# Gated linear attention and a two-stage mixer on one core: where the last two of six transpositions stand, and in which order ACT copies them

## What is computed

```python
m_new = max(f[t] + m, i[t]);  f_stab = exp(f[t] + m - m_new);  i_stab = exp(i[t] - m_new)
C = f_stab * C + i_stab * outer(v[t], k[t]);  n = f_stab * n + i_stab * k[t]
y[t] = sigmoid(o[t]) * (C @ q[t]) / max(abs(n @ q[t]), 1.0)
```

```python
h = relu(x.T @ w_tok1) @ w_tok2        # 768 -> 256 -> 768, over tokens
u = x + h.T
out = u + relu(u @ w_ch1) @ w_ch2      # 320 -> 1536 -> 320, over channels
```

## Time and profile before

| | us |
|---|---|
| median of 3 runs | 486.13 |
| lowest, highest | 482.44, 488.3 |
| the profiled execution, its own time | 481.5 |
| its span | 479.8 |
| PE, DVE, ACT, POOL busy | 451.7, 285.9, 227.6, 157.4 |

### The profile page before, as it was taken

How to read it: one execution, slowest core, us unless ns; L and a number is a source line. 1 busy time by engine, 2 the same in 40 slices (tenths; PEclk the granted TensorE clock), 3 DMA queues, 4 the chain that set the end, 5 groups by cost and what they waited for, 6 DMA issues and landing times.

```text
span 479.8 us, 9414 instructions
## 1 busy us (share of the span) xinstructions
PE 451.7 (94%) x3408; PEld 414.7 (86%) x3408; DVE 285.9 (60%) x660; ACT 227.6 (47%) x564; POOL 157.4 (33%) x212
## 2 busy tenths in 40 slices
PE   5988998788999999899999999899999999999996
PEld 3665787678999999789999999789999998899996
DVE  7476877777787425588787325587797324412312
ACT  2634557865655225865665125766555212212111
POOL 3424232546655001366655002266654000000000
PEclk9998799899999999999999999899999999999999
DMA  7499897224444302344454301344431001000101
GB/s 215 138 256 268 238 286 262 71 79 135 135 141 138 103 1 63 95 135 133 135 149 131 103 10 59 88 134 136 134 103 43 1 1 42 1 0 1 42 0 41
DMA packets 39189, 50.91 MB, mean 106 GB/s; under 512 B 3554, under 2 KB 31016, under 8 KB 39144
## 3 DMA queue, kind: packets, MB, share of 16 engines
q1 hardware_dynamic: 39144, 50.32, 35.2%
HBM read 46.27 MB, written 4.03 MB: 105 GB/s over the span
## 4 chain that ended last, share of the span: by engine, by line
PE 80%; ACT 6%; DVE 6%; issue 3%; DMA 3%; SPq 1%; POOL 0%; DVEq 0%; ACTq 0%; POOLq 0%
PE pC L952 30%; PE pA L1024 6%; PE pA L1025 6%; PE pA L1026 6%; PE pS L872 6%; PE pA L952 4%; PE pY L929 4%; PE pA L1028 3%; PE pA L1029 3%; DMA qd<-qT_dram 3%; PE pY L910 3%; PE pN L886 2%; PE pC L840 1%; DVE wc_lo L679 1%; PE pY L919 1%
## 5 line engine op out<-in xcount | busy, mean ns | idle before, releaser
L813 DVE SCALAR_TENSOR_TENSOR h_lo<-pA,h_hi 128x384 fp32r<-128x384 f32 x96 | 53.2, 554 | 119.0 <-ACT h_hi L615 119.0
L615 ACT ACTIVATE h_hi<-pA 128x384 fp32r<-128x384 f32 x96 | 46.7, 486 | 132.8 <-PE pA L1029 132.8
L952 PE MATMUL pC<-wc_hi,h_hi 128*128 128x320 f32 x288 | 94.0, 326 | 0.1
L952 PE MATMUL pC<-wc_lo,h_hi 128*128 128x320 f32 x288 | 89.0, 309 | 0.0
L952 PE MATMUL pC<-wc_hi,h_lo 128*128 128x320 f32 x288 | 88.6, 308 | 0.0
L422 POOL TENSOR_TENSOR gb<-gb,pb 128x384 f32<-128x384 f32 (+1 forms) x54 | 46.5, 862 | 112.1 <-ACT pb L529 111.9
L519 ACT ACTIVATE gb<-gb,aT 128x128 f32<-128x128 f32 x192 | 63.0, 389 | 14.3 <-POOL gb L433 14.3
L1024 PE MATMUL pA<-uT_hi,wc_hi 128*128 128x384 f32 x192 | 65.7, 342 | 2.5 <-DVE uT_hi L791 2.5
L1025 PE MATMUL pA<-uT_lo,wc_hi 128*128 128x384 f32 x192 | 65.0, 339 | 0.0
L1026 PE MATMUL pA<-uT_hi,wc_lo 128*128 128x384 f32 x192 | 64.7, 337 | 0.0
L952 PEld LDWEIGHTS pC<-wc_hi,h_hi 128*128 128x128 f32 x288 | 54.3, 189 | 0.9 <-issue 0.4
(11 more groups left out here) (113 smaller groups left out, 871.1 us busy)
## 6 DMA issues: line engine op xcount, KB each, us to landing
gb<-g_dram SPq DMA_DIRECT2D x23, 512.0 KB, 3.9
kv<-kvN_dram SPq DMA_DIRECT2D x24, 324.0 KB, 4.9
kd<-kT_dram SPq DMA_DIRECT2D x24, 180.0 KB
qz<-qT_dram SPq DMA_DIRECT2D x72, 60.0 KB
out_dram<-u SPq DMA_DIRECT2D x24, 160.0 KB, 1.9
gq<-g_dram SPq DMA_DIRECT2D x60, 60.0 KB
qd<-qT_dram SPq DMA_DIRECT2D x20, 180.0 KB, 5.1
x<-o_gate_dram SPq DMA_DIRECT2D x4, 640.0 KB, 4.5
```

The source lines that it names most:

```text
L615: nc.scalar.activation(h2[0][:, slot % 2], pA[slot % 2][:, 0:HALF], ACT.Relu).then_inc(h2_hi, 1)
L813: nc.vector.scalar_tensor_tensor(h2[1][:, slot % 2], pA[slot % 2][:, 0:HALF], 0.0, h2[0][:, slot % 2].bitcast(F32), ALU.max, ALU.subtract) ...
L952: ins = mm(dst, a[p], b[q], start=first and n == 0, stop=last and n == 2)
```

## The change

The last two transpositions (tiles 4 and 5) go to `pC[0]` and `pC[1]` instead of `pA`, and stand in slot 0: that of tile 4 behind the hidden product, that of tile 5 behind step 2 of the attention. Slots 0 and 1 wait for the low parts of tiles 2 and 3 only; the first `project` waits for all six. PE makes the second token product of tiles 0 to 2 with the piece `m` as the outer loop. Transposition 0 stands ahead of the products of tile 3, transposition 1 behind them, 2 behind tile 4's, and 3 behind tile 5's and step 1 of the attention.

ACT makes the high copy of tile `s - 2` behind its instruction for `u_twice` of tile `s`, where before it was that of tile `s - 1`. Step 1 of the attention moves behind tile 5 on all three engines. Relu of slot 0 stands ahead of the exponentials of step 3. The two last high copies, these exponentials, the start of the next tile (`chunk_start`) and `sigmoid` come between relu of slot 0 and that of slot 1. On DVE `p_low` of step 0 stands behind the low parts of tile 3, and the low parts of tiles 4 and 5 in slot 0.

```diff
...
@@ -148,6 +147,10 @@
         def scores_bank(ba, m):
             return [pS, pC[0], pC[1]][m % NG] if ba == 0 else pS
+
+        def transposed_bank(s):
+
+            return pA[s % 2] if s < NC - 2 else pC[s - (NC - 2)]
         def values_bank(ba, c):
@@ -589,23 +592,21 @@
                     nc.scalar.activation(h1[0][:, m], pA[m][:, 0:DM], ACT.Relu).then_inc(h1_hi, 1)
                 if more:
                     attention(b + 1, 0)
-                for s in range(NC + 1):
-                    if s < NC:
-                        act.wait_ge(u_ready, NC * b + s + 1)
-                        nc.scalar.activation(u[:, s, DM:3 * L], u[:, s, 2 * L:DM], ACT.Copy).then_inc(u_twice, 1)
-                    if s == 0:
-                        continue
-                    s -= 1
+                def u_high(s):
                     act.wait_ge(uT_mm, NC * b + s + 1)
-                    src = pA[s % 2][:, 0:3 * L].rearrange("p (t s) -> p t s", t=3)
+                    src = transposed_bank(s)[:, 0:3 * L].rearrange("p (t s) -> p t s", t=3)
                     nc.scalar.activation(uh[:, :, s * L:(s + 1) * L], src, ACT.Copy).then_inc(uT_hi, 1)
-                    if more and s + 1 == SECOND_AT:
-                        attention(b + 1, 1)
+
+                for s in range(NC):
+                    act.wait_ge(u_ready, NC * b + s + 1)
+                    nc.scalar.activation(u[:, s, DM:3 * L], u[:, s, 2 * L:DM], ACT.Copy).then_inc(u_twice, 1)
+                    if 2 <= s < NC - 1:
+                        u_high(s - 2)
                 if more:
-
+                    attention(b + 1, 1)
+                u_high(NC - 3)
+                if more:
                     p_middle(b + 1, AHEAD - 1)
-                    exps(b + 1, NG)
-                    chunk_start(b + 1, 1)
                 for slot in range(SLOTS):
                     k = SLOTS * b + slot
@@ -616,10 +617,17 @@
                     if b == 0:
                         for n in slot_pieces(slot):
                             split_hi(n)
-                    if more and slot == 0:
-                        sigmoid(b + 1)
+                    if slot == 0:
+                        u_high(NC - 2)
+                        if more:
+                            exps(b + 1, NG)
                     if more:
                         attention(b + 1, slot + AHEAD)
+                    if slot == 0:
+                        u_high(NC - 1)
+                        if more:
+                            chunk_start(b + 1, 1)
+                            sigmoid(b + 1)
             for b in range(B):
                 batch(b, b < B - 1)
@@ -786,9 +794,10 @@
                 def u_low(s):
...
+                    bank_s = transposed_bank(s)
+                    nc.vector.tensor_tensor(ul[:, :, cols], bank_s[:, 0:2 * L].rearrange("p (t s) -> p t s", t=2),
...
-                    nc.vector.tensor_tensor(uh[64:128, 2, cols], pA[s % 2][64:128, 2 * L:3 * L],
...
                 if more:
@@ -798,14 +807,13 @@
                     if b != 0:
                         dve.wait_ge(out_done[s // ST], 16 * ST * b)
                     nc.vector.tensor_tensor(u[:, s, 0:DM], pC[s % ST][:, 0:DM], x[:, s], ALU.add).then_inc(u_ready, 1)
-                    if s >= 2:
+                    if 2 <= s < NC - 1:
                         u_low(s - 2)
-                    if more and s == SECOND_AT:
-                        attention(b + 1, 1)
+                if more:
+                    attention(b + 1, 1)
+                u_low(NC - 3)
                 if more:
                     p_low(b + 1, 0)
-                for s in range(NC - 2, NC):
-                    u_low(s)
                 for slot in range(SLOTS + 1):
                     k = SLOTS * b + slot
                     if slot < SLOTS:
@@ -813,11 +821,15 @@
                         nc.vector.scalar_tensor_tensor(h2[1][:, slot % 2], pA[slot % 2][:, 0:HALF], 0.0,
                                                        h2[0][:, slot % 2].bitcast(F32),
                                                        ALU.max, ALU.subtract).then_inc(h2_lo, 1)
+                    if slot == 0:
+                        u_low(NC - 2)
                     if b == 0:
                         for n in slot_pieces(slot):
                             split_lo(n)
                     if more and slot < SLOTS:
                         attention(b + 1, slot + AHEAD)
+                    if slot == 0:
+                        u_low(NC - 1)
                     if slot == NJ or slot == SLOTS:
                         half = slot // NJ - 1
                         dve.wait_ge(c2_mm, SLOTS * b + slot)
@@ -974,38 +986,46 @@
                 def transposes(s):
+                    bank_s = transposed_bank(s)
                     pe.wait_ge(u_ready, NC * b + s + 1)
-                    if s >= 2:
+                    if s < 2:
+                        pe.wait_ge(h1_lo, MT * b + s + 1)
+                    elif s < NC - 2:
                         pe.wait_ge(uT_lo, 2 * (NC * b + s - 1))
-                    else:
-                        pe.wait_ge(h1_lo, MT * b + s + 1)
...
                     pe.wait_ge(u_twice, NC * b + s + 1)
...
                 if more:
                     attention(b + 1, 0)
-                for s in range(NC):
-                    if s < ST:
-                        if b != 0:
-                            pe.wait_ge(out_ready, 2 * ST * b)
-                    else:
-                        pe.wait_ge(u_ready, NC * b + s - ST + 1)
+                def mixed(s, m):
+
+                    return split_products(pC[s % ST][:, 0:DM], [w[:, m, s * L:(s + 1) * L] for w in wt2],
+                                          [a[:, m] for a in h1], m == 0, m == MT - 1)
+
+                if b != 0:
+                    pe.wait_ge(out_ready, 2 * ST * b)
+                for m in range(MT):
+                    pe.wait_ge(h1_lo, MT * b + m + 1)
+                    if b == 0:
+                        pe.wait_ge(w_lo, 2 + m + 1)
+                    for s in range(ST):
+                        ins = mixed(s, m)
+                        if m == MT - 1:
+                            ins.then_inc(t2_mm, 1)
+                transposes(0)
+                for s in range(ST, NC):
+                    pe.wait_ge(u_ready, NC * b + s - ST + 1)
                     for m in range(MT):
-                        if s == 0:
-                            pe.wait_ge(h1_lo, MT * b + m + 1)
-                            if b == 0:
-                                pe.wait_ge(w_lo, 2 + m + 1)
-                        ins = split_products(pC[s % ST][:, 0:DM], [w[:, m, s * L:(s + 1) * L] for w in wt2],
-                                             [a[:, m] for a in h1], m == 0, m == MT - 1)
+                        ins = mixed(s, m)
                     ins.then_inc(t2_mm, 1)
-                    if s >= 1:
-                        transposes(s - 1)
-                    if more and s == SECOND_AT:
-                        attention(b + 1, 1)
-                transposes(NC - 1)
+                    if s < NC - 1:
+                        transposes(s - 2)
+                if more:
+                    attention(b + 1, 1)
+                transposes(NC - 3)
                 def hidden(slot):
@@ -1014,7 +1034,9 @@
                     cols = slice(half * HALF, (half + 1) * HALF)
                     f = slice(j * L, (j + 1) * L)
                     if slot < 2:
-                        pe.wait_ge(uT_lo, 2 * (NC * b + NC - 1 + slot))
+                        pe.wait_ge(uT_lo, 2 * (NC * b + ST + slot))
+                    if half == 1 and j == 0:
+                        pe.wait_ge(uT_lo, 2 * NC * (b + 1))
                     if slot >= 2:
                         pe.wait_ge(h2_lo, k - 1)
                     if b == 0 and half == 0 and j % 6 == 0:
@@ -1033,6 +1055,8 @@
                     half, j = divmod(slot, NJ)
                     k = SLOTS * b + slot
                     pe.wait_ge(h2_lo, k + 1)
+                    if j == 0 and half == 0:
+                        pe.wait_ge(uT_lo, 2 * NC * (b + 1))
                     if j == 0 and half == 1:
                         pe.wait_ge(out_ready, 2 * ST * b + ST)
                     if b == 0 and half == 0 and j % 2 == 0:
@@ -1045,8 +1069,12 @@
                 for slot in range(SLOTS + 1):
                     if slot < SLOTS:
                         hidden(slot)
+                    if slot == 0:
+                        transposes(NC - 2)
                     if more and slot < SLOTS:
                         attention(b + 1, slot + AHEAD)
+                    if slot == 0:
+                        transposes(NC - 1)
                     if slot >= 1:
                         project(slot - 1)
```

7 lines of the change are left out of this document (3 added, 4 removed).

## The result

The changed kernel took 495.9 us (median of 4 runs, 493.69 to 497.0), the kernel before 484.28 beside it (480.46 to 488.3). The ratio is 1.0271, with a 95% interval of 1.0217 to 1.0325: **slower by 2.7%**, as forecast. The forecast was 495.0, in a range of 482 to 501.

The account below looks back on a forecast made before the run. PE, with 80% of the chain, was taken to bound the kernel, time being won or lost in its waits at the borders. Delays of 4.2 + 2.9 + 1.6 + 0.1 = 8.8 us on a 486.13 median gave 495.0, range 482 to 501.

Parts of the forecast that it names:

- The ring: Loop over tiles: each addition from tile 3 on waits for an older tile's high copy; 2.01 us a tile, before 1.22.
- The wait of PE for `p_low` in slot 0: Second border, after slot 0's hidden product: PE waits some 2 us for p_low, needed for step 2's values.
- The chain to relu of slot 1: ACT's and DVE's work up to relu of slot 1: 4.2, 2.9 and 1.6 us later at the first three borders.
- That a delay there is passed on in full: Behind slot 2's wait PE is busy without a gap, so 4.2, 2.9 and 1.6 us count whole at three borders.
- half clock: Rival: PE falls to half clock more often, 1.6 us behind each of three borders, 499.7 us; chance 0.16.
- The last part, where I forecast 0.1: Last border, no attention: nine products cover h1's low half, the ring costs 2.4; first project 0.1 us later.
- the 8.8 of the sum: Delays at the four borders added: 4.2 + 2.9 + 1.6 + 0.1 = 8.8 us.
- the first two rivals: Ring does not bind and banks help, 480.9 us, chance 0.14; ACT's queue does not reach PE, 487, chance 0.22.
- The first: Rival: ring does not bind, banks remove PE's waits at second, third and last border; 5.2 us gain, 480.9; chance 0.14.

Follow-up runs that it names:

- ring open: Changed kernel with ACT's high copy of tile s - 1, not s - 2, behind u_twice of tile s; 487.08 us, ratio 1.0084 to the kernel before.
- the fillers: Changed kernel with products that nobody reads put into PE's waits at the borders; 494.8 us, ratio 1.0194 to the kernel before.
- the banks alone: Kernel before with transpositions of tiles 4 and 5 into pC and fewer waits, all instructions in their old place; 477.7 us, ratio 0.9890; again 478.58, 0.9880.
- moving one call: Changed kernel with only the sigmoid moved ahead of step 2 of the attention; 491.84 us, ratio 1.0158 to the kernel before.
- ring and step 1 mended: Changed kernel with high copy of s - 1, step 1 back behind tile 3, and here the sigmoid ahead of step 2; 483.12 us, ratio 0.9959.
- step 1 back: Changed kernel with step 1 of the next attention back behind tile 3 on PE, ACT and DVE; 491.81 us, ratio 1.0154 to the kernel before.
- ring with step 1: Changed kernel with high copy of s - 1 behind u_twice of s and step 1 back behind tile 3; 485.13 us, ratio 1.0095.
- PE's order: Kernel before with the banks and the change's PE order up to tile 5, transpositions 4 and 5 right behind tile 5; 481.25 us, ratio 0.9981.

## Why the prediction was right

**The ring.** Forecast 2.01 us a tile, measured 1.98; slot 0 8.9 behind the first product, measured 9.1. I had put the first product of before at 184.26 by counting back from the earlier trace rows, while it starts at 183.96: from there my forecasts are 9.2 for slot 0 and 19.5 for relu of slot 1 (measured 19.54). Opening the ring took 6.3 us of 11.5 away, about 1.0 of it clock at the last border. The wait of PE for `p_low` in slot 0 came too (1.73 us, some 2 forecast), but it is step 0's values that it holds up and not step 2's, as I wrote. The Trainium skill, "TensorE: Matmul & The Clock Gate", section "Architectural detail: the array is 16× 32×32, not 1× 128×128", has ACT and DVE take their instructions strictly in order; the trace agrees, as ACT idles 1.34 us in each turn with a high copy next in line whose tile PE had long transposed.

**The chain to relu of slot 1.** Forecast delays of relu of slot 1 behind the first product: 4.2, 2.9 and 1.6 us at the first three borders; measured 4.24, 2.92 and 1.69 (21.69, 19.54 and 19.53 against 17.45, 16.62 and 17.84). This step was right to a tenth of a microsecond, since every duration in it came from a row and every order from the program.

**That a delay there is passed on in full.** The intervals grew by 4.4, 3.9 and 1.9. So nothing was taken up, and at the second border 1.0 was added. The stretches of 86.1 to 86.9 us behind step 2's values show the same for the second and third border in 12 executions.

**The term that was mis-sized** is half clock, which I had at nothing in the sum and as a rival of 1.6 us a border. Behind the second border it cost about 1.0 (87.5 us behind step 2's values in place of 86.1 to 86.9): PE's products in slot 1's project at 215 us follow each other by 0.27 us in place of 0.15. Behind the third it fell ahead of PE's waits and cost nothing (that part is 110.4, and 110.3 with the fillers). The last part, where I forecast 0.1, grew by 1.2, of which 1.0 is half clock: with the same code there it is 76.8 and 77.0 in the two executions in which the clock fell, and 75.8 and 75.9 in the two in which it held. The fillers took 1.8 away in all. Added to the 8.8 of the sum, some 2 make 10.8 of the 11.5 measured. Both of the cases, my forecast and this rival, were partly true; the first two rivals are out for the change. The first, which I priced at 5.2 us of gain, is near to what the banks alone gave (1.1%, or 5.3 us by the ratio). I also misread how often the clock fell before: not at one border of four but at two, the first of them at 91 us, behind a wait of PE of 1.82 us.

```profile
91.00:93.00 2.00, 1.97 (x14) 0.53 0.03 8
```

**What I did not see** is the place of the sigmoid. I had summed ACT's work between the relus rightly, wait for the scores included, but took the wait as given. It is there only because the sigmoid no longer stands ahead of it. In the sum it made no difference; for the cause it does, since moving one call starts step 2's values in slot 2 0.7 us sooner, and 1.0 with ring and step 1 mended, and the clock then holds behind them. In the batches that is 3.1 us (4.0 less the 0.9 of the last border) and 5.6.

**The base.** I forecast from 486.13, the median then known. Beside the changed kernel the kernel before had 484.28, and in 17, 19 and 23 runs on other chips 483.44, 482.0 and 482.48. So the change cost more than my 8.8, some 11 to 13 us, and that the forecast of 495.0 came within 1 us of 495.9 is in part luck: a base that was 2 to 4 us high made up for the half clock that the sum left out.

## What to carry to other kernels

Where two engines hand tiles to each other, write down for each instruction what it stands behind on its own engine, and look for a closed loop: a delay of one place in one list (high copy of `s - 2` behind `u_twice` of `s`) turned a pipeline of 1.2 us a tile into a ring of 2.0. Long work that nobody waits for, such as a table load with its sigmoid, did better here ahead of a wait than behind it; look then where the next table load falls. And a change of several parts is worth taking apart: one part of this one, the two banks, was a gain of 1.1% by itself (3.8 us in the batches), hidden under a loss four times as large.

## What the runs showed of the hardware

The head is the same program in all 13 profiled executions of the table, and took 67.6 to 75.8 us. It goes with the granted clock: from 60 to 68 us this was 1.00 for the heads of 67.6 to 69.2, 0.86 and 0.51 for the two of 71.1 and 71.8, and 0.50 to 0.67 for those of 73.3 to 75.8. So where the stretches at the lower level fall goes with a difference of 8 us, 1.7% of the whole. A low clock between 40 and 60 us does not go with it: it was 0.65 and 0.83 there in two stretches of 10 us with a head of 68.7, and 1.00 and 0.97 with one of 73.6. For changes of 1% the cut at the borders told more than the medians did.

The clock fell behind waits of 1.2 and 1.8 us that followed each other in slot 2, in all six places at the second and third border where both stood (the changed kernel, ring open, step 1 back, and ring with step 1), and stayed up when these were filled. A single wait of 1.6 us in slot 2 lowered it in none of six places (the banks alone, twice, and with PE's order). In between it went both ways, with the same waits in one and the same execution: 0.7 and 1.8 us, and a single one of 2.19, lowered it at the second border and not at the third. So waits of PE tell how likely a fall is, not whether it comes.

What a fall costs depends on what follows. Ahead of a wait it cost nothing (the changed kernel, third border), and behind the last wait of a border 0.7 to 2.2 us.
